# Straight blocks and the loop's first block in one order, and the next block's transposes between two halves of a second product

## The reference

```python
def reference(**kwargs):
    attn_out = _attn_ref(**attn_kwargs)          # r, k, v (4, 8, 768, 48)
    x = attn_out.transpose(0, 2, 1, 3).reshape(B * S, H * D)      # 3072 x 384
    x = _moe_ref(x=x, **moe_kwargs)              # 384 -> 2048 -> 384
    return _moe2_ref(x=x, **moe2_kwargs)

def _moe_ref(x, w_in, w_out):
    h = x @ w_in
    return np.maximum(0.01 * h, h) @ w_out

def _moe2_ref(x, w_skip, w_gate, w1, w2):        # E = 8, F = 1024
    do_compute = x @ w_skip > 0
    xc = x[do_compute]
    e_idx = np.argmax(xc @ w_gate, axis=1)
    ...
    for e in range(E):
        mask = e_idx == e
        h = np.maximum(xc[mask] @ w1[e], 0.0)
        y[mask] = gate_w[mask, None] * (h @ w2[e])
    out[do_compute] = xc + y
```

## Time and profile before

| | us |
|---|---|
| median of 3 runs | 679.3 (678.01 to 679.57) |
| profiled execution | 678.46 |
| its span, first to last instruction | 676.6 |
| TensorE busy | 648.1 (96%) |
| VectorE busy | 401.7 (59%) |
| ScalarE busy | 309.6 (46%) |
| GpSimd busy | 80.2 (12%) |
| mean granted clock of TensorE | 0.992 |

### The profile page before, as it was taken

The page is one execution under the profiler, slowest core; times in us unless marked ns, Lnnn a source line. Parts: engine busy times, 40 slices in busy tenths (PEclk is TensorE's granted clock), DMA queues, the critical chain, the costliest instruction groups (busy, mean ns, idle before and its releaser), DMA issues.

```text
span 676.6 us, 14123 instructions
## 1 busy us (share of the span) xinstructions
PE 648.1 (96%) x4733; PEld 608.4 (90%) x4734; DVE 401.7 (59%) x864; ACT 309.6 (46%) x682; POOL 80.2 (12%) x102
## 2 busy tenths in 40 slices
PE   8889999999999999999999999999998899999982
PEld 7778899999999999999999999999998789999982
DVE  8866665646656465566456554743477645947740
ACT  4475534445334444344443444434356245837630
POOL 5140000100010001001000100010030322223210
PEclk9999999999999999999999999999999999999997
DMA  8936625220422321242204222004214278593300
GB/s 223 296 119 206 210 70 173 72 70 15 135 66 70 112 67 45 60 141 71 66 16 138 67 70 94 13 13 166 93 57 154 94 246 291 190 355 136 119 11 6
DMA packets 39324, 78.08 MB, mean 115 GB/s; under 512 B 9032, under 2 KB 27494, under 8 KB 39216
## 3 DMA queue, kind: packets, MB, share of 16 engines
q1 hardware_dynamic: 34272, 62.96, 29.7%
q10 hardware_dynamic: 2432, 9.76, 4.2%
q0 software_dynamic: 2560, 4.58, 2.1%
HBM read 61.68 MB, written 13.00 MB: 110 GB/s over the span
## 4 chain that ended last, share of the span: by engine, by line
PE 87%; DVE 4%; ACT 3%; DMA 2%; issue 2%; POOL 1%; SPq 0%; DVEq 0%; ACTq 0%; POOLq 0%
PE bank L798 30%; PE bank L818 28%; PE bank L1004 8%; PE bank L965 7%; PE bank L663 3%; PE bank L725 3%; PE bank L732 2%; DMA const<-in_consts 2%; PE bank L987 2%; PE bank L746 1%; PE bank L876 1%; ACT am L1073 1%; PE bank L888 1%; DMA rkt<-in_rk_t 1%; DVE w_lo L1508 1%
## 5 line engine op out<-in xcount | busy, mean ns | idle before, releaser
L1417 DVE TENSOR_TENSOR h_sb<-h_sb,bank 128x384 f32<-128x384 f32 x128 | 70.8, 553 | 159.2 <-ACT h_sb L1111 159.2
L1111 ACT ACTIVATE h_sb<-bank 128x384 f32<-128x384 f32 x128 | 62.8, 491 | 221.8 <-PE bank L798 221.6
L798 PE MATMUL bank<-x_hi,win_hi 128*128 128x384 f32 x384 | 135.0, 352 | 1.3 <-DVE win_lo L1462 0.9
L818 PE MATMUL bank<-wout_hi,g_hi 128*128 128x394 f32 x384 | 131.9, 343 | 1.5 <-DVE state L1393 1.5
L818 PE MATMUL bank<-wout_hi,g_lo 128*128 128x394 f32 x384 | 131.2, 342 | 0.0
L818 PE MATMUL bank<-wout_lo,g_hi 128*128 128x394 f32 x384 | 131.1, 341 | 0.0
L798 PE MATMUL bank<-x_hi,win_lo 128*128 128x384 f32 x384 | 129.4, 337 | 0.0
L798 PE MATMUL bank<-x_lo,win_hi 128*128 128x384 f32 x384 | 129.2, 336 | 0.0
L1424 DVE TENSOR_TENSOR g_lo<-h_sb,g_hi 128x384 fp32r<-128x384 f32 x128 | 71.6, 559 | 30.9 <-ACT g_hi L1118 29.9
L1118 ACT ACTIVATE g_hi<-h_sb 128x384 fp32r<-128x384 f32 x128 | 66.8, 522 | 47.7 <-DVE h_sb L1417 46.5
L798 PEld LDWEIGHTS bank<-x_hi,win_hi 128*128 128x128 f32 x384 | 72.1, 188 | 8.6 <-issue 6.1
(11 more groups left out here) (244 smaller groups left out, 890.1 us busy)
## 6 DMA issues: line engine op xcount, KB each, us to landing
raw<-in_experts SPq DMA_DIRECT2D x32, 768.0 KB, 6.0
rkt<-in_rk_t SPq DMA_DIRECT2D x46, 192.0 KB, 3.8
rkn<-in_rk_nat SPq DMA_DIRECT2D x21, 384.0 KB, 4.3
v<-in_v_nat SPq DMA_DIRECT2D x24, 192.0 KB, 2.9
z_rows<-z_sb SPq DMA_DIRECT2D x24, 192.0 KB, 2.8
out<-z_sb SPq DMA_DIRECT2D x24, 192.0 KB, 2.9
stage<-in_win ACTq DMA_DIRECT2D x4, 768.0 KB, 4.5
stage<-in_wout_t ACTq DMA_DIRECT2D x4, 768.0 KB, 6.4
```

The costliest lines, as they stand in the source:

```text
L798: mm = pe.matmul(h_ps[t % 2][:, 0:GT], a[:, kk, cols], b[G % 2][:, kk, :], start=n == 0, stop=n == 3 * KT - 1)
L818: mm = pe.matmul(z_ps[i][:, 0:ZW], a[t % 3][:, tok], b[:, f, :], start=f == 0 and j == 0, stop=f == FT - 1 and j == 2)
L1111: act.activation(h_sb[t % 2][:], h_ps[t % 2][:, 0:GT], ACT.Copy, scale=SLOPE).then_inc(s_h_scaled, 1)
L1417: dve.tensor_tensor(h_sb[t % 2][:], h_sb[t % 2][:], h_ps[t % 2][:, 0:GT], ALU.max).then_inc(s_leaky, 1)
```

## The change

1. TensorE's order at the seam: block 1's transposes stand between the halves of block 0's second product; the loop's first rows are turned after half of block 1's second product, two slices of it stand before the loop's first product and the last two behind that. The transposes of the loop's block 0 stand ahead of the loop.
2. In the loop the transposes of block j+1 stand between the two halves of block j's second product. Their high and low parts (`eht_of`) are kept in two pairs of tiles, by the block's parity.
3. The first straight product waits for its own block's rows alone (`i + 1` for `AHEAD`).
4. The three pieces of the straight blocks' second weights are spread: ScalarE does one before the last hidden copy, the others after the turned rows; VectorE does one after each block's turned rows and the third after the picks.
5. VectorE does the low parts of straight block 0 before the last steps of the plan, and those of block 1 right after the list of ids, ahead of `id_put`. In the loop it does the low parts of block j+1 ahead of the add of block j.
6. GpSimd gathers the rows of the loop's block 0 with a spot, `first_spot`, that VectorE writes where it chooses the order of the experts, and reads the plan after that.
7. ScalarE waits for the second product of the block before, ahead of the first piece of new second weights. The straight block 1's second product writes bank 6 in place of bank 2.

```diff
@@ first_product_a
-                pe.wait_ge(s_zt_a_lo, AHEAD)
+                pe.wait_ge(s_zt_a_lo, i + 1)
@@ TensorE, behind the steps
             first_product_a(1, (2,))
-            second_product_a(0, 0)
-            second_product_a(0, 1)
+            second_product_a(0, range(0, 4))
             turn_hidden_a(1)
-            second_product_a(1, 0)
-            turn_first_rows()
-            second_product_a(1, 1)
...
+            second_product_a(0, range(4, 8))
+            second_product_a(1, range(0, 4))
+            pe.wait_ge(s_plan_done, 1)
             blocks = pe.value_load(plan[0:1, TOTAL:TOTAL + 1], min_val=E, max_val=BLOCKS)
+            pe.wait_ge(rows_in[0], 16)
+            turn_rows(0)
+            second_product_a(1, range(4, 6))
             pe.wait_ge(s_w1_lo, PIECES)
             pe.wait_ge(s_zt_lo, 1)
             first_product(0, 0)
+            second_product_a(1, range(6, 8))
             pe.wait_ge(rows_in[1], 16)
             turn_rows(1)
-            pe.wait_ge(s_res_a, AHEAD)
+            pe.wait_ge(s_relu_done, 1)
+            turn_hidden()
@@ TensorE, a block of the loop
                             cur, odd, _, _, nxt, nxt_odd = entries(pe, regs, j)
-                            pe.wait_ge(s_relu_done, j + 1)
-                            for f in range(EFT):
-                                mm = pe.transpose(eht_ps[f // 4][:, P * (f % 4):P * (f % 4) + P],
-                                                  eh[:, P * f:P * f + P], ident)
-                            mm.then_inc(s_eht_done, 1)
...
+                            if u == 1:
+                                pe.wait_ge(s_res_a, AHEAD)
+                            pe.wait_ge(s_eht_lo, 2 * j + 1)
+                            pe.wait_ge(s_w2_lo, PIECES * cur + PIECES)
+                            second_product(u % 2, odd * EW, 0)
                             pe.wait_ge(s_eht_lo, 2 * j + 2)
...
+                            with pe.If(j < blocks - 1):
+                                pe.wait_ge(s_relu_done, j + 2)
+                                turn_hidden()
+                            second_product(u % 2, odd * EW, 1)
@@ ScalarE
+                if step == STEPS - 3:
+                    high_w2_early(0, (0,))
                 if step + 2 < STEPS:
                     high_g(step + 2)
...
                     turned_rows_a(step + AHEAD - STEPS)
-                if step == STEPS - 2:
-                    high_w2_early(0)
+                    high_w2_early(0, (step + AHEAD - STEPS + 1,))
...
                             with act.If(new > 0):
+                                act.wait_ge(s_ey_done, j)
                                 act.wait_ge(s_w2_in, e + 2)
@@ VectorE
+                dve.tensor_scalar(first_spot[:], hot_at[:], float(TILES), float(AHEAD), ALU.mult,
+                                  ALU.add).then_inc(s_order, 1)
...
             route_a(GROUPS - 1)
+            low_w2_early(0, (2,))
             route_gates(GROUPS - 1)
...
             turned_rows(0, 1)
+            low_w2_early(1, range(PIECES))
             add_rows_a(1)
             turned_rows(1, 2)
-            low_w2_early(1)
+            for half in range(2):
+                dve.wait_ge(s_eht_hi, half + 1)
+                turned_hidden(0, half)
...
                                 low_w2(e, odd, range(1, PIECES))
+                            with dve.If(j < blocks - 1):
+                                for half in range(2):
+                                    dve.wait_ge(s_eht_hi, 2 * j + half + 3)
+                                    dve.sem_inc(s_dve_past, 1)
+                                    turned_hidden((u + 1) % 2, half)
                             dve.wait_ge(s_ey_done, j + 1)
@@ GpSimd
+            reg = pool.alloc_register("pool_spot")
+            pool.load(reg, first_spot[0:1, 0:1])
+            spot_0 = pool.snap(reg, min_val=0, max_val=SPOTS - 1)
             pool.wait_ge(s_z_store, 16 * 2 * TILES)
+            pool.wait_ge(s_spots, 1)
+            pick_ids(0, spot_0)
+            gather(0, 0)
             pool.wait_ge(s_plan_done, 1)
             blocks = pool.value_load(plan[0:1, TOTAL:TOTAL + 1], min_val=E, max_val=BLOCKS)
```

More of the change, by code:

```diff
@@ L867, in turn_hidden_a, with second_product_a @@
                         mm.then_inc(s_eht_a_done, 1)
-            def second_product_a(i, half):
-                pe.wait_ge(s_eht_a_lo, 2 * i + half + 1)
+            def second_product_a(i, parts):
+                pe.wait_ge(s_eht_a_lo, 2 * i + parts[-1] // 4 + 1)
                 pe.wait_ge(s_w2_lo, PIECES)
-                for f in range(4 * half, 4 * half + 4):
+                for f in parts:
                     for a, b in ((eht_a_hi, w2_hi), (eht_a_hi, w2_lo), (eht_a_lo, w2_hi)):
@@ L889, in turn_rows, with first_product, turn_hidden, second_product @@
                 mm.then_inc(s_zt_done, 1)
[L891 to L895, removed]
+            def first_product(par, base):
+                for kk in range(KT):
+                    for a, b in ((zt_hi, w1_hi), (zt_hi, w1_lo), (zt_lo, w1_hi)):
+                        for c in range(2):
+                            mm = pe.matmul(eh_ps[c][:], a[par][:, kk, :],
+                                           b[:, bass.ds(base + EF * kk + 512 * c, 512)],
+                                           start=kk == 0 and a is zt_hi and b is w1_hi,
+                                           stop=kk == KT - 1 and a is zt_lo)
+                mm.then_inc(s_eh_done, 1)
+            def turn_hidden():
+                for f in range(EFT):
+                    mm = pe.transpose(eht_ps[f // 4][:, P * (f % 4):P * (f % 4) + P],
+                                      eh[:, P * f:P * f + P], ident)
+                    if f % 4 == 3:
+                        mm.then_inc(s_eht_done, 1)
+            def second_product(par, base, half):
+                for f in range(4 * half, 4 * half + 4):
+                    hi, lo = eht_of[par]
+                    for a, b in ((hi, w2_hi), (hi, w2_lo), (lo, w2_hi)):
+                        mm = pe.matmul(ey_ps[par][:, 0:DM], a[:, f, :], b[:, bass.ds(base + DM * f, DM)],
+                                       start=f == 0 and a is hi and b is w2_hi,
+                                       stop=f == EFT - 1 and a is lo)
+                if half:
+                    mm.then_inc(s_ey_done, 1)
             pe.wait_ge(s_kn_clear, 1)
@@ L1151, in turned_rows_a, with high_w2_early @@
                                ACT.Copy).then_inc(s_zt_a_hi, 1)
-            def high_w2_early(e):
+            def high_w2_early(e, pieces):
                 act.wait_ge(s_h_done, STEPS)
                 act.wait_ge(raw1_load[e], 64)
-                for i in range(PIECES):
+                for i in pieces:
                     cols = slice(EW * e + PIECE * i, EW * e + PIECE * i + PIECE)
@@ L1501, in turned_rows_a, with low_w2_early @@
                                   ALU.subtract).then_inc(s_zt_a_lo, 1)
-            def low_w2_early(e):
-                for i in range(PIECES):
+            def low_w2_early(e, pieces):
+                for i in pieces:
                     cols = slice(EW * e + PIECE * i, EW * e + PIECE * i + PIECE)
```

63 lines of the change are left out of this document (23 added, 40 removed).

## The result

The changed kernel takes 673.29 us (median of 7 runs, 672.39 to 674.72) against 679.57 (677.45 to 682.76): 0.9916 of the time, 95% interval 0.9894 to 0.9937, so 4.3 to 7.2 us less. The forecast was 673.0. The profiled execution took 673.93 with a span of 672.2. A second time, beside other kernels, the ratio was 0.9926 (0.9903 to 0.9949).

The account below looks back on a forecast made before the run. TensorE, busy 96% of the span, was taken as the bound, so only its stops and slow clock could be won. Seam 2.9, loop 0 and tail 3.4 made 6.3 us off 679.3: 673.0, range 670.3 to 676.0.

Parts of the forecast that it names:

- First straight product: Straight part's start: waiting only for its own block's rows, TensorE loses the whole stop of 2.05 us.
- Rank: Matmuls ranking the last tokens: new TensorE wait of 0.2 us for VectorE's picks, bounds 0 and 1.2.
- Routing chain 0.9 earlier: VectorE's slot step at the seam moves from 526.27 to 525.4; rival that the chain keeps its time: chance 0.09.
- Block 1's straight second product: Seam: new wait of 0.2 us on VectorE's subtraction behind the id list, bounds 0 and 0.98.
- The gather: Loop's first rows: TensorE waits 1.7 us for them, the largest new wait, bounds 0.8 and 2.6.
- Low half of the first rows: Loop's first rows, from turning to usable low half: 0.2 us left uncovered.
- Into the loop: Loop's entry: stop of 0.85 on the relu goes; TensorE's plan read costs a new 0.5 us, bounds 0 and 1.2.
- Sum of the seam: Last project matmul to block 1's first loop product: 5.65 us of stops less 2.8 of new waits, gain 2.85.
- The loop: Blocks keep 9.52 us each; cost 0, bounds 0 and 1; TensorE feels ScalarE only when 1.3 us late.
- The tail: Last first product to last scatter: 15.6 us instead of 19.07, wait 0.5 instead of 2.21, no slow clock; gain 3.4.
- the clock did not fall at the new wait: Rival: clock falls at the new stop of 1.7 us, costing 1.8 more, 674.8 us; chance 0.12.
- The slower case: Rival: ScalarE late in the six weight-making blocks, TensorE waits for each relu, priced at 682 us; chance 0.04.

Follow-up runs that it names:

- e8: Changed kernel with TensorE's plan read a block ahead, routing chain shortened, second block's rows turned before the straight product's last two slices; 671.28 us, 0.9894 of before.
- e1: Kernel before with the loop's new order alone; straight part, its weight pieces and first gather as before; 1.0016 of before.
- e6: Changed kernel with VectorE's third weight piece behind the last tokens' destinations and the id list ahead of the plan's last steps; 0.9904 of before.
- e7: Changed kernel with GpSimd's reads of the plan put ahead of the first gather again; 0.9936 of before.
- e9: Changed kernel with two pieces of a block's second weight converted ahead of the relu instead of one; 0.9919 of before.
- e5: Kernel before with sixteen matmuls whose result nobody reads ahead of the last block's second product; 1.0056 of before.
- e5b: Kernel before with four matmuls whose result nobody reads ahead of the last block's second product; 0.9978 of before.
- e2: Kernel before with the new straight part, its weight pieces and early first gather alone; loop as before; 0.9955 of before.
- e10: Kernel before with the loop's new order alone, plus TensorE's plan read a block ahead; 0.9969 of before.

## Why the prediction was right, and where it was not

The time, the sign and the mechanism held: stops of TensorE went, and a smaller one on the gather came. Term by term, with times after less 0.71 to set them on before's clock:

- *First straight product*: right, no bracket at 521.36; and the piece that ScalarE does earlier cost nothing, as forecast. *Rank*: forecast 0.2, measured 0.16.
- *Routing chain 0.9 earlier*: the slot step came 4.80 behind the last project matmul (525.98), 5.80 before; 1.0. The id list was forecast for 534.9 to 535.2 and came at 534.8, the gather for 536.3 and came at 536.3:

```profile
535.49 0.25 DVE L1798 TENSOR_SCALAR id_get<-found 128x192 uint32<-128x192 f32 x1
```

```profile
537.01 1.00 POOL L1959 DMA_INDIRECT zg<-z_rows,get  x1 [0.83 <-POOL get L1954]
```

- *Block 1's straight second product*: forecast 0.2, measured none; the half was ready at 536.31, TensorE came at 536.57.
- *The gather*: forecast 1.7, measured 1.25 in the bracket. I counted from the start of the last matmul plus 0.175, which makes 1.42 here; TensorE also came about 0.2 later than I had it. *Low half of the first rows*: 0.2 and 0.20.
- *Into the loop*: forecast 0.5, measured 1.14; **the term that was mis-sized most**. I let the transposes cover the read and took the register steps to lie beside it. But the read stands behind the transposes in the sequencer's order, and behind the steps that enter the loop (from 547.4), so it began at 548.0, when the transposes (from 547.45) were more than half done, and the register steps come behind the read. The rows of TensorE's queue (count: ns min/median/max, first and last start):

```profile
L997 PEldq MOVE  x1: 33/33/33, 547.4 to 547.4; - x1
...
L465 PEldq TENSOR_LOAD <-plan x1: 885/885/885, 548.0 to 548.0; - x1
```

It ended at 548.9; the weights of block 1's product were loaded at 549.62. So 0.6 of steps into the loop and 0.7 of register steps were left out; e8 shows that all but 0.1 of the stop can be hidden.

- *Sum of the seam*: the new waits were forecast as 2.8 and are 2.75, by errors that cancel (0.2 and 0.45 too much, 0.64 too little). The gain is 2.50 and not 2.85: I charged the 0.17 of lost overlap to the stops that go, but not to the four that come; with it the sum would have been 2.2. The other 0.3 is a stop of before without a bracket, at the loop's entry: the transposes end at 551.32 (550.23 + 1.09) and the product starts at 551.42, 0.1 of idle and 0.17 of overlap.
- *The loop*: costed at 0, measured 0.47, inside the bound of 1 but not for the reason that I bounded. ScalarE was never felt. The cost is one stop, with its lost overlap, where the loop first returns to its top. The read there began 1.6 ahead of the first product (586.6 to 588.25), in the next block 2.4 (595.5 to 597.87), at the second return 1.9 (624.5 to 626.40), and read and register steps need 1.6:

```profile
L465 PEldq TENSOR_LOAD <-plan x1: 839/839/839, 586.6 to 586.6; - x1
...
L465 PEldq TENSOR_LOAD <-plan x1: 817/817/817, 595.5 to 595.5; - x1
...
L465 PEldq TENSOR_LOAD <-plan x1: 817/817/817, 624.5 to 624.5; - x1
```

So a return brings the read 0.5 later and the first one 0.8; what makes the first later than the second is not shown. In five more profiles with this read at the first return (the second of the changed kernel, e1, e6, e7, e9) the stop is 0.13 to 0.23. Before, the read of that block began 2.3 ahead of the transposes that follow it (586.5 to 588.80), and they did not wait.

- *The tail*: 15.6 forecast, 15.94 measured; wait 0.65 for 0.5 (0.24 of issue stands between the subtraction and the product), clock at 1.00 as forecast, product 4.44 for 4.2 (the last matmul's end and the lost overlap). That GpSimd's chain ends close behind held: e9 runs into it at 15.11.
- *Rivals*: the clock did not fall at the new wait; the condition was real, as e7 shows with a stop of 2.35; what a stop of the forecast's 1.7 would have done, no run shows. The routing chain did gain its 0.9. The slower case did not come: the latest relu is 0.95 late, against 1.6 before, so the step that ScalarE gets its pieces relatively earlier held; e9 puts the cover at the 1.3 of the forecast. The chances of the cases called faster add up to 0.94, not 0.93.
- *The total*: forecast 6.3 from the trace, measured 5.16; 678.46 - 5.16 + 0.71 is 674.0, and the profiled execution took 673.93. The medians differ by 6.28 and the ratio says 5.7, so the median came out at the forecast although the trace's gain is 1.1 smaller: that 673.0 was met within 0.3 is partly luck. Part of the difference is that before's runs spread over 5.3 us and after's over 2.3. The granted clock of every run is on record: beside the experiments the kernel before ran 60 times, in 25 of them with a mean clock of 0.990 or less (median 679.7), in 35 with more (677.4); the changed kernel had 0.990 or less in 2 of 12 runs. Before's profile, with the one fall at the tail, has 0.992, the changed kernel's, with none, 0.994. So a lower clock was more frequent in before. Falls behind its long stops, as in e5, would make it so, but where the clock fell in runs without a profile is not shown.

## What to carry to other kernels

When an order is rewoven, list what each engine's sequencer does between the instructions: a read of a few words into registers and the steps behind it took TensorE's sequencer 1.6 us here, and a loop's entry or return some more ahead of it; this is free as long as enough matmuls are queued ahead of it and in the open as soon as a wait stands just before. Price a stop by its length and by the clock behind it: where the clock fell behind a stop of 2.05 to 2.35 us, that cost 0.9 to 1.6 us on top of its length (e7, e5, e5b against before). Two changes with gains of their own may share a cost; e2 and e10 add up only once the read is out of the way.

## What the hardware showed

- The same stop of 2.05 us between the same matmuls left the granted clock at 1.00 in four profiles (before, e1, e5b, e10) and was followed by 0.50 in a fifth (e5: 4.57 for 3.02 us of matmuls).
- A stop of 2.35 between matmuls was followed by a clock of 0.50 in the one profile that has it (e7); stops of 1.2 to 1.4 at the same place left it at 1.00 in five.
- TensorE's read of six words of the plan took 0.81 to 0.89 us in its queue in the changed kernel; ScalarE's and VectorE's of eight took 0.55 and 0.60 (medians).
